# Attention and two expert layers on one core: a shorter opening, gate products that stream both input halves at once, and an earlier end of GpSimd's program

## The reference

```
scores = scale * q @ k.T            # 4 batches, 8 heads, 576 tokens, head size 64, window of 64 keys
x = softmax(mask(scores)) @ v       # 2304 tokens x 512
gate = sigmoid(x @ w_gate); val = x @ w_val        # 512 -> 1536
x = (gate * val) @ w_out                            # 1536 -> 512
noisy = x @ w_gate2 + log1p(exp(x @ w_noise)) * noise   # 8 experts, top 2 of them
out[rows of e] += weight * (relu(x @ w1[e]) @ w2[e])    # 512 -> 1024 -> 512
```

## Time and profile before

| | us |
|---|---|
| median of three runs | 1001.63 |
| the profiled execution's own time | 1001.99 |
| its span, from the first instruction to the last | 1000.3 |
| TensorE busy in the span | 980.6 (98%) |
| VectorE, ScalarE, GpSimd busy | 441.0, 368.6, 337.0 |

### The profile page before, as it was taken

The page is one execution under the profiler, slowest core; times in us unless marked ns, Lnnn a source line. Parts: engine busy times, 40 slices in busy tenths (PEclk is TensorE's granted clock), DMA queues, the critical chain, the costliest instruction groups (busy, mean ns, idle before and its releaser), DMA issues. The chain is left out here.

```text
span 1000.3 us, 18621 instructions
## 1 busy us (share of the span) xinstructions
PE 980.6 (98%) x7173; PEld 894.1 (89%) x7173; DVE 441.0 (44%) x1207; ACT 368.6 (37%) x906; POOL 337.0 (34%) x317
## 2 busy tenths in 40 slices
PE   7999999999999999999999999999999999999994
PEld 6999899999999999999999899898998989898983
DVE  4663454453535445353445535444434344444410
ACT  5553343424333343332344423333424233343410
POOL 3781023021201212120112324563827273745211
PEclk9999999999999999999999999999999999999997
DMA  6664235243334424330234242772736464564312
GB/s 214 213 191 127 87 120 148 66 138 107 117 95 129 125 60 132 107 104 18 103 106 138 43 137 45 188 167 72 160 76 149 105 149 111 140 133 111 57 18 35
DMA packets 82970, 113.55 MB, mean 114 GB/s; under 512 B 19264, under 2 KB 45888, under 8 KB 82880
## 3 DMA queue, kind: packets, MB, share of 16 engines
q1 hardware_dynamic: 69104, 84.76, 28.2%
q0 software_dynamic: 13344, 27.05, 14.1%
q10 hardware_dynamic: 432, 0.52, 0.2%
HBM read 83.52 MB, written 28.77 MB: 112 GB/s over the span
## 5 line engine op out<-in xcount | busy, mean ns | idle before, releaser
L897 PEld LDWEIGHTS bank<-xr,wr 128*128 128x128 f32 x2592 | 324.8, 191 | 9.6 <-issue 0.8
L897 PE MATMUL bank<-xr,wr 128*128 128x256 f32 x2592 | 327.6, 283 | 0.4 <-issue 0.4
L998 PE MATMUL bank<-wr 128*128 128x256 f32 (+1 forms) x1536 | 223.8, 307 | 0.6 <-DVE wr L1575 0.4
L998 PEld LDWEIGHTS bank<-wr 128*128 128x128 f32 x1536 | 221.3, 190 | 2.1 <-DVE wr L1575 0.7
L718 POOL DMA_INDIRECT arena<-x_rows,shared x120 | 130.9, 1091 | 143.6 <-DVE v_nat L1562 95.3
L914 PE MATMUL bank<-wr,hr 128*128 128x512 f32 x648 | 172.3, 401 | 0.0
L1446 DVE SCALAR_TENSOR_TENSOR arena<-arena,bank 128x256 f32<-128x256 f32 x108 | 45.5, 421 | 201.9 <-ACT arena L1184 201.7
L1014 PE MATMUL bank<-wr 128*128 128x512 f32 (+1 forms) x576 | 133.2, 391 | 0.0
L914 PEld LDWEIGHTS bank<-wr,hr 128*128 128x128 f32 x648 | 114.4, 189 | 20.8 <-issue 0.2
L1184 ACT ACTIVATE arena<-bank 128x256 f32<-128x256 f32 x108 | 41.4, 383 | 246.9 <-PE bank L897 246.8
L1014 PEld LDWEIGHTS bank<-wr 128*128 128x128 f32 (+1 forms) x576 | 105.0, 184 | 24.6
(11 more groups left out here) (143 smaller groups left out, 742.1 us busy)
## 6 DMA issues: line engine op xcount, KB each, us to landing
arena<-moe_w SPq DMA_DIRECT2D x40, 512.0 KB, 4.4
arena<-moe_w SPq DMA_DIRECT2D x96, 128.0 KB, 4.8
p_rows<-arena SPq DMA_DIRECT2D x28, 256.0 KB, 2.8
v_nat<-p_rows SPq DMA_DIRECT2D x112, 64.0 KB
arena<-gv SPq DMA_DIRECT2D x12, 512.0 KB, 4.2
out<-zeros POOLq DMA_DIRECT2D x20, 256.0 KB, 4.3
x_rows<-arena SPq DMA_DIRECT2D x9, 512.0 KB, 4.4
arena<-v SPq DMA_DIRECT2D x34, 128.0 KB, 4.0
```

The lines of the kernel that those rows point to most:

```text
L897: mm = pe.matmul(o, gv_w[:, f, w, kk], xr[:, g % 2, x, kk], start=(m + kk + n == 0), stop=(kk == KC - 1 and n == 2), skip_group_check=True)
L998: mm = pe.matmul(ps_h[u % 2][:, 0:n], w1_r[e % 2][:, a, kk, f * P:(f + 1) * P], xT[p][:, b, kk, 0:n], start=(kk + x == 0), stop=(kk == KC ...
```

## The change

Four things. First, in the opening: both halves of q's and k's second tile are loaded ahead of v; block 0 reads its values from `v_nat`, and block 2 its from two tiles already there, in two half sets of 64 rows (`values(2)` has 16 products instead of 8), so that two loads go; idle products are moved and fewer; and GpSimd waits for the four `scale_first` before its first two splits of `w_out`. Second, in the steps of groups 1 to 7 (`wide`, 84 of 108 steps) a high weight tile is loaded once and streams both input halves, 512 columns, into a whole bank; the low weight tile streams 256 columns, as before. Gate and value have a bank each now, every step the same two. The two halves of a bank are added by VectorE, `add_gates` and `add_vals`, and the rest reads the sums from SBUF. Third, `h_low` of these steps goes to GpSimd, ahead of `scale`, and GpSimd's transfers for placing rows and for zeroing stand at other steps. Fourth, GpSimd reads the count of left-over tiles ahead of its last two scatters and doesn't wait for these; SyncE does.

```diff
+        def wide(c):
+            return FC <= c < LAST - FC
+        def row_of(c):
+            return 0 if wide(c) else c % 2
...
             def load_v(t):
                 if t:
-                    sp.wait_ge(pv_done, 2 * t if t > 2 else 2)
+
+                    sp.wait_ge(pv_done, 2 * t if t > 2 else 3)
...
             sp.dma_start(kT[:, 2], k[0, :, 1]).then_inc(k_in[0], 16)
-            load_mixed(0)
+            load_k(1)
+            load_q(1)
             load_v(0)
-            load_k(1)
             load_first()
...
-            load_mixed(1)
+            load_mixed(2)
             load_v(2)
-            load_mixed(2)
...
+            for u in range(2):
+                sp.wait_ge(scattered[u], 16 * scatters(ALL, u))
...
+            def h_low(c):
+                r = c % 2
+                pool.wait_ge(h_hi, c + 1)
+                pool.tensor_tensor(hr[:, r, 1], gate[:, 0], hr[:, r, 0].bitcast(F32), ALU.subtract).then_inc(h_lo, 1)
...
+            pool.wait_ge(scaled_first, OPEN)
             split_out(0)
             split_out(1)
             for s in range(LAST):
+                if wide(s):
+                    h_low(s)
...
+                if m == ALL - 2:
+                    count = left_count(pool)
...
-            for u in range(2):
-                pool.wait_ge(scattered[u], 16 * scatters(ALL, u))
-            left_tiles(pool, left_rows)
+            def added():
+                for u in range(2):
+                    pool.wait_ge(scattered[u], 16 * scatters(ALL, u))
+            left_tiles(pool, left_rows, count, added)
...
-                if c >= 2:
-                    pe.wait_ge(h_done, c - 1)
-                else:
-                    pe.wait_ge(masked, OPEN - 1)
                 for m in range(2):
-                    o = ps_g[f % 2][:, m * GT:(m + 1) * GT]
+                    if c == 0:
+                        pe.wait_ge(masked, OPEN - 1)
+                    elif wide(c - 1):
+                        pe.wait_ge(vals_added if m else gates_added, c - FC)
+                    else:
+                        pe.wait_ge(h_done if m else gate_done, c)
                     for kk in range(KC):
-                        for n, (w, x) in enumerate(((m, 0), (m, 1), (2 + m, 0))):
-                            mm = pe.matmul(o, gv_w[:, f, w, kk], xr[:, g % 2, x, kk], start=(m + kk + n == 0),
-                                           stop=(kk == KC - 1 and n == 2), skip_group_check=True)
-                mm.then_inc(gv_done, 1)
+                        if wide(c):
+                            pe.matmul(ps_g[m].rearrange("p (a n) -> p a n", a=2), gv_w[:, f, m, kk], xr[:, g % 2, :, kk],
+                                      start=(kk == 0), stop=False, skip_group_check=True)
...
+                        mm = pe.matmul(ps_g[m][:, 0:GT], gv_w[:, f, 2 + m, kk], xr[:, g % 2, 0, kk], start=False,
+                                       stop=(kk == KC - 1), skip_group_check=True)
+                    mm.then_inc(gv_done if m else gates_up, 1)
...
+            def add_gates(c):
+                dve.wait_ge(gates_up, c + 1)
+                dve.wait_ge(h_lo, c)
+                dve.tensor_reduce(gate[:, 0], ps_g[0].rearrange("p (a n) -> p n a", a=2), AX.X, ALU.add).then_inc(gates_added, 1)
+
+            def add_vals(c):
+                dve.wait_ge(gv_done, c + 1)
+                dve.wait_ge(h_done, c)
+                dve.tensor_reduce(gate[:, 1], ps_g[1].rearrange("p (a n) -> p n a", a=2), AX.X, ALU.add).then_inc(vals_added, 1)
```

More of the change, by code:

```diff
@@ L397, in unit, with left_count, left_tiles @@
             return w1_r[e % 2][:, x, n] if n < KC else w2_r[:, x, 2 * (n - KC):2 * (n - KC) + 2].rearrange("p f n -> p (f n)")
-        def left_tiles(eng, step):
+        def left_count(eng):
             eng.wait_ge(left_done, 1)
-            n = eng.value_load(more_i[0:1, 2, 0:1], min_val=0, max_val=MORE - 1)
+            return eng.value_load(more_i[0:1, 2, 0:1], min_val=0, max_val=MORE - 1)
+        def left_tiles(eng, step, count=None, first=None):
+            n = left_count(eng) if count is None else count
             with eng.If(n > 0):
+                if first is not None:
+                    first()
                 with eng.Fori(0, n) as r:
@@ L440, in mixed @@
         def mixed(t):
-            return sum(1 if starts(2 * n) else 2 for n in range(t + 1))
+            return sum(1 if starts(2 * n) else 2 for n in range(2, t + 1))
         def stage(s, offset, late):
@@ L686, in constants, with place_rows @@
                                    pattern=[[1, P]], channel_multiplier=-1).then_inc(consts2, 1)
[L688 removed]
+            def h_low(c):
+                r = c % 2
+                pool.wait_ge(h_hi, c + 1)
+                pool.tensor_tensor(hr[:, r, 1], gate[:, 0], hr[:, r, 0].bitcast(F32), ALU.subtract).then_inc(h_lo, 1)
+            def place_rows(g, some=range(2 * CH)):
                 pool.wait_ge(tab_filled, 16)
@@ L693, in place_rows @@
                 pool.nop(nofuse=True)
-                for t in range(2 * g, 2 * g + 2):
-                    for c in range(CH):
-                        pool.indirect_dma_start(places[:, :], bass.IndirectOffsetOnAxis(slot_i[:, t, c:c + 1], 0),
-                                                pairs[:, t, c], None).then_inc(placed if g < EARLY else placed_late, 16)
+                for i in some:
+                    t, c = 2 * g + i // CH, i % CH
+                    pool.indirect_dma_start(places[:, :], bass.IndirectOffsetOnAxis(slot_i[:, t, c:c + 1], 0),
+                                            pairs[:, t, c], None).then_inc(placed if g < EARLY else placed_late, 16)
             def gather(n):
@@ L753, in _ @@
                                        ).then_inc(pads_zeroed, 16)
-                if (g := at_slot(s, FC, 2 * FC + 2, EARLY)) is not None:
-                    place_rows(g)
+                for i in range(2 * CH):
+                    if (g := at_slot(s, FC, 2 * FC + 2 + i, EARLY - 1)) is not None:
+                        place_rows(g, [i])
+                if s == 2 * FC + 2 + FC * (EARLY - 1):
+                    place_rows(EARLY - 1)
                 if s == LAST - 8:
@@ L873, in values @@
                 pe.nop(nofuse=True)
-                rows = v_nat1 if n == 3 else v_nat if n % 2 else v_mix
+                if n == 2:
+                    for rows, r0, r1 in ((v_nat1, 0, WIN), (v_nat, WIN, P)):
+                        if r0:
+                            pe.wait_ge(half_done, 1)
+                        for c in range(GP):
+                            i, j = divmod(c, 2)
+                            for h in range(2):
+                                mm = pe.matmul(ps_x(n)[h * HD:(h + 1) * HD, c * WIN:(c + 1) * WIN],
+                                               rows[r0:r1, (2 * c + h) * HD:(2 * c + h + 1) * HD],
+                                               pT[r0:r1, 2 * i + h, j * WIN:(j + 1) * WIN], start=(r0 + c == 0), stop=(r0 > 0),
+                                               skip_group_check=True)
+                        mm.then_inc(pv_done if r0 else half_done, 1)
+                    return
+                rows = v_nat1 if n == 3 else v_nat if n % 2 or n == 0 else v_mix
                 for c in range(GP):
@@ L1028, in _ @@
             scores(1)
+            idle(3)
             scores(2)
-            idle(5)
+            idle(1)
             turn_p(0)
@@ L1033, in _ @@
             values(0)
-            idle(3)
+            idle(1)
             turn_p(1)
@@ L1190, in h_high @@
                     act.wait_ge(hr_used, c - 1)
-                act.copy(hr[:, r, 0], gate[:, r]).then_inc(h_hi, 1)
+                act.copy(hr[:, r, 0], gate[:, row_of(c)]).then_inc(h_hi, 1)
             def y_copy(g):
@@ L1598, in _ @@
                 g, f = divmod(s, FC)
+                if wide(s):
+                    add_gates(s)
+                    add_vals(s)
                 if 0 <= s < LAST:
@@ L1602, in _ @@
                     sums(n)
-                if 0 <= s < LAST:
+                if not wide(s):
                     h_low(s)
```

43 lines of the change are left out of this document (29 added, 14 removed).

## The result

| | before | after |
|---|---|---|
| median of the runs, us | 1001.59 (1000.98 to 1002.09, 4 runs) | 989.59 (989.49 to 989.89, 4 runs) |
| profiled execution: own time, span | 1001.99, 1000.3 | 989.6, 987.8 |

The ratio is 0.9881, with a 95% interval of 0.9864 to 0.9898: 12.0 us faster. The prediction was 986.2 us, with a range from 982.5 to 991.5. The direction, the place of the three large gains and the range held. The forecast's own range, 983.5 to 988.5, did not: 989.59 lies in the part that was added for the rivals. Two terms were off: the wide streams gave 3.6 us, where 6.8 were taken and 5.0 was the lower bound, and the last group gave 0.3 where it was to cost 0.2.

A forecast was written before the change was run, and what follows sets the result against it. TensorE, busy 98% of the span, was taken as the bound. 1001.99 - 6.8 (wide streams) - 4.2 (opening) - 4.6 (end) + 0.2 (last group) = 986.6 profiled, 986.2 us median; range 982.5 to 991.5, own range 983.5 to 988.5.

The forecast's parts named there:

- the wide streams: Gate products of 84 steps in groups 1 to 7: eight products fewer a step, saving 6.8 us (bounds 5.0 and 8.1).
- the last group: Narrow steps of the last group: gate products now wait for the tanh of the step before, costing 0.2 us.
- the first reason for the opening: Opening: q and k there at about 7, so third scores no longer wait until 8.92 and TensorE's idle pause goes.
- The rival of the waiting drain: Program's end: GpSimd's drain begins only at the landing, gain 1.4 instead of 4.6 us, 989.4 us in all; chance 12%.
- some 0.8 late into the next step, and the cover of 1.8 takes it: Step with the slots: 0.95 us more VectorE work comes 0.8 us late, hidden by a plain step's 1.8 us cover.
- The rival that was built on 2.5 ns: Wide streams: each product costs 2.5 ns, not 13, so gain 1.7 instead of 6.8 us, 991.3 us; chance 8%.
- The reductions, `h_low` and VectorE's load: Wide steps: reductions 0.69 us each, `h_low` on GpSimd 0.7, VectorE busy 2.9 of 4.7 us a step; nothing on the path.
- The rival in which VectorE bounds the groups: Groups 1 to 7: reductions of 1.75 us make each step 0.25 us longer, 1014 us in all; chance 3%.
- Moving `h_low` away ends that collision: Wide steps: VectorE's subtraction, 1.02 instead of 0.43 us while GpSimd scales, no longer collides with it.
- The opening: Before the loop: ScalarE carries the chain without its 4.01 us idle; loop begins at 18.75, not 22.94, saving 4.2 us.
- The rival in which GpSimd's splits hold the opening: Opening: GpSimd's two splits follow without a gap, `split_low(0)` and `x_low` come behind both; 988.8 us; chance 12%.
- The end: Behind the last send: GpSimd drains as soon as the send is done, ending at 995.5, saving 4.6 us.

The follow-up runs named there:

- e5: Changed kernel with VectorE's small router operations of `weights` one step later than those of `slots`; 988.59 us, groups 1 to 7 in 398.0 us.
- e1: Changed kernel with no wide step: every gate product has 256 columns, VectorE makes all low parts; 992.86 us, groups 1 to 7 in 402.65 us.
- e4: Changed kernel with each half's wide products reordered: four of 512 columns, then four of 256, instead of in turn; 988.02 us.
- e9: Changed kernel with products ordered so long and short change only twice a step; 987.46 us, groups 1 to 7 in 396.6 us.
- e12: Changed kernel with two-change product order, router weights one step later and q's second tile on ScalarE's queue; 986.79 us, groups 1 to 7 in 395.1 us.
- e7: Changed kernel with each `add_vals` done twice, one after the other; 995.79 us, groups 1 to 7 in 404.4 us.
- e6: Changed kernel with `h_low` of the wide steps back on VectorE; 989.63 us, groups 1 to 7 in 399.2 us.
- e11: Changed kernel with v's first tile loaded ahead of k's second again and q's second tile on ScalarE's queue; 990.90 us, loop starts at 18.85.
- e8: Changed kernel without GpSimd's branch for left-over tiles, the reading of the count kept; 991.22 us, on another chip than most runs.
- e2: Changed kernel with the end as before: GpSimd waits for its last scatters, then reads the count and ends; 993.90 us.

## Why the prediction was right, and where a term was off

The three gains came where the prediction put them, and by the mechanisms that it gave for them, but for the first reason for the opening. That the time lies in the stated range is in part luck: the term of the streams missed its own bounds (5.0 and 8.1), and the range reached as far as 991.5 only for rivals. The rival of the waiting drain had named 989.4, 0.2 us from what was measured, and its mechanism is not the one that happened.

**The wide streams: right in place, mis-sized.** The term was "I take 229, 2.789, 0.081 saved: x 84 = 6.8 us". The block takes 2.81 in the plain step, and without the late gate sum (e5) groups 1 to 7 took 397.97 us, 4.7 less than the 402.65 of e1: 0.056 saved a step. The error is in carrying the spacing of products that stand among their like (227 to 231.7) to a stream in which long and short alternate; the rows showed only unmixed ones, and the 231.7 of the earlier trace rows, six long products behind 24 short ones, was already the sign that the neighbour matters. e4 and e9 show it: the same products cost less the fewer the changes, and with fourteen long ones in a row and eight short ones (e12) the saving is 7.6 us, 0.090 a step, above the 0.081 that was taken. The other 1.0 us is the gate sum behind slots (e5). The prediction saw this step ("some 0.8 late into the next step, and the cover of 1.8 takes it") and applied the wrong cover: the 1.8 us belong to the chain from the value sum to the output products. The gate sum also frees the bank that TensorE asks for first in the next step, and there the count "1.4 + 1.39 us later" held only if VectorE was free when the sum came due. 4.7 - 1.0 comes to the 3.6 that groups 1 to 7 gained (402.65 - 399.01).

**The price per product.** The settled spacing is 227 ns for 512 columns and 120 for 256. The difference, 107 ns for 256 columns, is one column a cycle at the granted 2.4 GHz, and it leaves 13 ns that go with each product, as the prediction had it. The Trainium skill (TensorE: Matmul & The Clock Gate, Back-to-back issue gap) gives 2.5 ns for the isolated product, and says itself that in a stream of weight loads and products both set the spacing. No stretch of this kernel shows 2.5 ns, and the measurement decides. The rival that was built on 2.5 ns would have saved 1.7 us; the streams alone saved 4.7.

**The reductions, `h_low` and VectorE's load: right.** 0.69 us as worked out, 0.74 for 0.7, and VectorE busy for 2.98 us a step (250.33 / 84) for 2.9. The rival in which VectorE bounds the groups is out: with another 0.69 us a step (e7) a plain step doesn't move.

**"Moving `h_low` away ends that collision": true and worth nothing** (e6).

**The opening: right, 4.33 for 4.2, by its chain.** The reason given ahead of the chain was partly wrong: it put the early k and q first, and e11 finds 0.24 us in the order of v and k, which is within the scatter of that start. Most of the gain lies in the shorter wait for k and, with the larger part, between the third scores and the first turn, where idle products at the lower clock had stood. The rival in which GpSimd's splits hold the opening fell: `split_low(0)` took 2.24 us, until 17.26 and inside the bounds named, yet `x_low(3)` waited for ScalarE's last cast and not for VectorE. Both inputs of `split_low` and of GpSimd's subtraction stand in SBUF. The later `split_low` took 1.28 us, and GpSimd's subtraction took this in the kernel before, where VectorE ran nothing of the kind beside it:

```profile
13.17 1.27 POOL L661 TENSOR_TENSOR wr<-arena,wr 128x512 fp32r<-128x512 f32 x1
```

When they met (2.24 and 2.14 in the rows above) each took nearly twice as long. The Trainium skill (SBUF — State Buffer, SBUF: two separate sides) says that they exclude each other, and the rows agree.

**The last group: wrong sign, small.** The +0.2 us came from a tanh that would be late for the gate products. It was read at its old place, behind the value products. Now the gate has its own semaphore, set half-way through the products, and tanh can start before the value products are through:

```profile
506.33 0.38 ACT L1248 ACTIVATE arena<-bank 128x256 f32<-128x256 f32 x1
...
506.81 1.55 PE L976 MATMUL bank<-wr,hr 128*128 128x512 f32 x6
```

It starts ahead of the output products, and its bank is wanted only behind these. The 0.3 us gained are in one step, in which TensorE went over to turning rows (at 528.35 before) 0.27 us sooner. What it had waited for there isn't shown; e1, without wide steps, has the gain too, so it doesn't come from these.

**The end: right, 4.3 for 4.6.** The drain ended at 987.19, 5.75 us behind the send; 0.56 us lie between it and the span's end, for which 0.2 had been counted, and 0.24 in the four runs that have about 9.03 in the table. The rival in which the drain waits for the landing is out, since 984.7 + 5.75 would be 990.5 and the span ended at 987.8.

## What to carry to other kernels

When products of two lengths share a stream, group those of one length: the saving per product is only there in full behind some five long ones in a row. When a bank is freed by a reduction instead of by the last user, list every asker of that bank and check the cover at the step where the reducing engine is busiest, not in the plain one. And in this program the 5.75 us of GpSimd's end begin when GpSimd's own list is through, so whatever GpSimd does after its last send (here the waits and the count, 4.3 us) comes on top unless another engine can do it.

## What the runs showed of the hardware

- Spacing of products with a weight tile of 128x128 each at a granted clock of 1.00, by their position (e9): long behind short 233, 236, 228, 233, 231, then 227; short behind long 114, 119, then 120 ns. In strict alternation (after): 234 and 117 in the mean.
- GpSimd's drain ends 5.75 us behind the end of the last send where nothing stands behind this, with the branch (after) or without (e8), and over 2 us behind the landing. Where GpSimd first waits for the landing and reads the count (e2), it takes as long from there: 5.75 us from 986.0.
- A reduction of 128x512 to 128x256 that reads PSUM with a stride of 256 elements takes 0.69 us, on the line through the sizes 128x64 (0.22) and 128x320 (0.49) that read SBUF.
- A `tensor_tensor` of VectorE (128x1024) and one of GpSimd (128x512), each with both inputs in SBUF, take 2.24 and 2.14 us when they meet, where 1.28 and 1.27 are their times alone.
